# Experts and feed-forward in one block, output copies ahead of the logarithm, late weight pieces split in other steps

## The chip, the cores and the metric

The program runs on one core of one Trainium2 chip. The time is the device time of one execution in microseconds (us). A core has five engines with instruction queues of their own: TensorE (PE: matrix products and transposes; its weight loads are listed as PEld), VectorE (DVE), ScalarE (ACT), GpSimd (POOL) and SyncE (SP), which here issues nearly all data transfers.
## The reference

```python
x = attention(q, k, v)          # causal, window 128, linear bias; 4 x 576 tokens, 8 heads x 64
x = moe(x, w_skip, w_gate, w1, w2)   # top expert of 8; x + gate * (relu(x @ w1[e]) @ w2[e])
h = x @ w_in                    # 2304 x 512 times 512 x 2048
sp = np.where(h > 20.0, h, np.log1p(np.exp(np.minimum(h, 20.0))))
g = h * np.tanh(sp)
return (g @ w_out).astype(np.float32)   # 2304 x 2048 times 2048 x 512
```

## The kernel before

Three parts follow each other, each in a block of its own: `attention`, `experts` and `feed_forward`. At a block's end every engine waits for all others before it goes into the next block. `feed_forward` takes SBUF and PSUM only after `experts` has given its own back.

**Experts.** Tokens that go to the same pair of experts are gathered by GpSimd from `tokens` in DRAM, 128 rows (a job) at a time, and written back the same way. Of one job, `one` on TensorE does the hidden products (L1046), transposes and output products (L1064) into `ps_y`; VectorE's `scale_y` (L975) makes `y_sb`, and GpSimd's `put` (L763) scatters it. Behind the last job TensorE waits for `y_scaled` and does 20 warming products (`keep_warm`, L84 and L1093, two passes each); VectorE has six weight pieces of the feed-forward to split (`low_parts`, L961); GpSimd waits for its last scatter (L816). Weights are split because each product is made from three: the float32 matrices are held as a high part (`hi`, rounded) and the rest (`lo`), as are tokens and activations.

**Feed-forward.** The 2304 tokens are taken in six chunks of 384 (three tiles of 128). Each chunk has 16 steps, one for each 128 columns of the 2048 hidden ones. `step` exists once for each engine and is written out by hand; the order of the calls in it is the order on the engine. In step f:

- TensorE does `hidden` of step f (12 products, L1366) and then `output` of step f - 3 (9 products, L1383, into three PSUM banks `ps_o`, one for each token tile, over all 16 steps). So the last `output` of a chunk stands in step 2 of the next, and the first of the next chunk in its step 3.
- VectorE caps the hidden values (`u_sb`, L1313), makes `g` of step f - 2 (`n_sb`, L1317), two operations for step f - 1 (L1322, L1324), and the polynomial `n_sb` of step f (L1330).
- ScalarE takes an exponential (L1264), rounds `g` to `g_hi` (L1270), takes a logarithm (L1275) and a second exponential (L1277).
- GpSimd makes `g_lo` (L1236), for which `output` waits, and the ratio (L1230).

In steps 3, 6, 9 and 12 (`AHEAD`) TensorE also transposes a quarter of the next chunk (L1352), ScalarE rounds it to `xt_hi` (L1258) and VectorE makes `xt_lo` (L1304). In chunk 0, eight late weight pieces of 256 columns are split too: `SPLIT` gives for ScalarE's step f the piece whose high part it makes (L1284), and VectorE makes its low part one step later (L1338). When a chunk's last `output` is done, ScalarE copies the three banks to `o_sb` (L1292), at the end of that step; SyncE stores them (L1204). TensorE's first `output` of the next chunk waits for the copy of each bank.

The first tokens come by three loads (L1208), one for each tile, at the start of the block, followed by the two late weight loads (L1210). TensorE transposes them as they arrive (L1403), into `ps_o` and `ps_xt`.

Of the kernel before, what the change touches and what calls it, by code (L numbers as in the profile page):

```python
# [24 lines left out]
P = 128  # L25
# [546 lines left out]
def experts(nc, ctx, dram, ffn, cst):  # L572
# [8 lines left out]
    FB = F1 // P  # L581
    w_sb = sb("w_sb", [P, 4 * KD * F1])
# [81 lines left out]
    block = ctx.enter_context(nc.Block())  # L664
# [43 lines left out]
    def _(sp):  # L708
# [11 lines left out]
        for p in range(2, PH):  # L720

            done = jobs_of(sp, p - 2)
            sp.wait_ge(y_ready[p - 2], done)
# [4 lines left out]
    def _(pool):
# [87 lines left out]
        pool.wait_ge(y_scattered[PH - 1], before * 16)  # L816

# [177 lines left out]
    def _(pe):  # L995
# [96 lines left out]
        pe.wait_ge(y_scaled[PH - 1], totals[PH - 1])  # L1092
        keep_warm(nc, ps_y[0], cst, 20)  # L1093

def feed_forward(nc, ctx, dram, ffn, cst, out):
# [19 lines left out]
    SPLIT = {f: f - 1 for f in range(1, 1 + MINI)}  # L1116
# [43 lines left out]
    block = ctx.enter_context(nc.Block())  # L1160
# [35 lines left out]
    def _(sp):  # L1196
# [54 lines left out]
    def _(act):  # L1251
# [8 lines left out]
        def step(c, f, par):  # L1260
# [4 lines left out]
            if t2.exists():  # L1265
# [4 lines left out]
                nc.scalar.activation(g_hi[:, t2.r], n_sb[:, t2.f % NB], ACT.Copy).then_inc(g_hi_ready, 1)  # L1270
            if t.exists():
# [14 lines left out]
            if o.exists() and o.f == FT - 1:  # L1286

                for i in range(CT):
                    act.wait_ge(*((o_ready, o.c * (CT - 1) + i + 1) if i < CT - 1 else (g_used, o.s + 1)))
                    if i == 0 and (not isinstance(o.c, int) or o.c >= 1):  # L1290
                        act.wait_ge(o_stored, o.c * 16)
                    nc.scalar.activation(o_sb[:, i], ps_o[i][:, :], ACT.Copy).then_inc(o_copied, 1)  # L1292
# [120 lines left out]
def program(nc, dram, out):  # L1413
    with ExitStack() as ctx:
# [86 lines left out]
```

## Time and profile before

| | us |
|---|---|
| Median of three runs | 819.0 |
| Lowest and highest | 814.56, 819.47 |
| The profiled execution | 817.42 |
| Its span, first to last instruction | 815.6 |
| TensorE, VectorE, ScalarE, GpSimd busy | 782.9, 497.4, 366.0, 352.3 |
| Feed-forward, first transposes to the end | 377.2 to 815.6 |

The times below are in us from the start of the span. In a timeline, a row of several equal instructions (x3) gives their common length; what stands in brackets is how long the engine had been idle before and what ended this. The ends of matrix products are modelled, so a product that follows another closely starts before the other's listed end.

### The profile page before, as it was taken

To read this page: it belongs to the slowest core of one execution; us is meant where nothing else is said; L and a number is where in the kernel's file an instruction comes from. 1 tells how busy PE (TensorE), PEld (TensorE's weight loads), DVE (VectorE), ACT (ScalarE), POOL (GpSimd) and SP (SyncE) were. 2 spreads that over 40 slices of the span, in tenths; PEclk is the share of its full clock that TensorE was granted. 3 is DMA by queue.
4 is the path that set the end of the run, shared out by engine and by line. 5 is a ranking of instruction groups with operands and counts; after the bars stand their busy time and mean duration, and the time that the engine had idled before them with its cause. 6 is when DMAs were issued, how large, how long until landed. Compare 5 with 4: busy or idle time off the path is not lost.

```text
span 815.6 us, 13948 instructions
## 1 busy us (share of the span) xinstructions
PE 782.9 (96%) x4708; PEld 594.2 (73%) x4708; DVE 497.4 (61%) x878; ACT 366.0 (45%) x881; POOL 352.3 (43%) x447
## 2 busy tenths in 40 slices
PE   8999999998999999997899999999999999999996
PEld 4787788877333333337788898888888988888995
DVE  3666666665111111334888878777877787786784
ACT  4667777620101010442554545555454445455443
POOL 3555555511111021000455556555655655565654
PEclk9999999999999999998999999999999999999999
DMA  5566888610789175004001010110100001001001
GB/s 201 173 187 190 287 274 262 194 39 16 258 291 341 62 280 204 8 14 134 0 1 40 0 40 0 39 40 1 40 21 17 5 33 39 0 0 40 0 1 40
DMA packets 50325, 77.78 MB, mean 95 GB/s; under 512 B 22083, under 2 KB 23363, under 8 KB 50240
## 3 DMA queue, kind: packets, MB, share of 16 engines
q1 hardware_dynamic: 48656, 72.19, 26.8%
q0 software_dynamic: 1600, 4.70, 1.5%
q8 instruction: 40, 0.66, 0.3%
q14 instruction: 29, 0.24, 0.1%
HBM read 65.36 MB, written 12.32 MB: 95 GB/s over the span
## 4 chain that ended last, share of the span: by engine, by line
PE 42%; DVE 5%; issue 3%; ACT 1%; POOL 1%; DMA 0%; POOLq 0%; SPq 0%; ACTq 0%; DVEq 0%
PE ffn_h L1366 21%; PE ffn_o L1383 20%; DVE n_sb L1330 1%; POOL n_sb L1230 1%; DVE u_sb L1313 1%; DVE ffn_lo L1338 1%; DVE n_sb L1317 1%; DVE u_sb L1322 1%; PE ffn_xt L1352 1%; ACT r_sb L1275 1%; DMA x_sb<-tokens 0%; POOL g_lo L1236 0%; ACT o_sb L1292 0%; DVE r_sb L1324 0%; ACT xt_hi L1258 0%
## 5 line engine op out<-in xcount | busy, mean ns | idle before, releaser
L1236 POOL TENSOR_TENSOR g_lo<-n_sb,g_hi 128x384 fp32r<-128x384 f32 x96 | 119.7, 1247 | 179.4 <-ACT g_hi L1270 179.4
L1230 POOL TENSOR_TENSOR n_sb<-n_sb,r_sb 128x384 f32<-128x384 f32 x96 | 125.5, 1307 | 20.6 <-DVE r_sb L1324 20.6
L1366 PE MATMUL ffn_h<-xt_hi,ffn_lo 128*128 128x384 f32 x384 | 132.9, 346 | 0.5 <-DVE xt_lo L1304 0.5
L1275 ACT ACTIVATE r_sb<-n_sb,all_consts 128x384 f32<-128x384 f32 x96 | 59.3, 618 | 164.1 <-DVE n_sb L1330 164.1
L1366 PE MATMUL ffn_h<-xt_lo,ffn_hi 128*128 128x384 f32 x384 | 130.7, 340 | 0.0
L1366 PE MATMUL ffn_h<-xt_hi,ffn_hi 128*128 128x384 f32 x384 | 130.7, 340 | 0.0
L1383 PE MATMUL ffn_o<-ffn_hi,g_lo 128*128 128x512 f32 x288 | 116.0, 403 | 13.1 <-POOL g_lo L1236 7.0
L1330 DVE SCALAR_TENSOR_TENSOR n_sb<-u_sb 128x384 f32<-128x384 f32 x96 | 125.8, 1311 | 1.5 <-ACT u_sb L1264 1.5
L1383 PE MATMUL ffn_o<-ffn_lo,g_hi 128*128 128x512 f32 x288 | 114.5, 397 | 0.0
L1383 PE MATMUL ffn_o<-ffn_hi,g_hi 128*128 128x512 f32 x288 | 113.6, 395 | 0.0
L1313 DVE TENSOR_SCALAR u_sb<-ffn_h 128x384 f32<-128x384 f32 x96 | 53.2, 554 | 48.1 <-PE ffn_h L1366 48.1
L366 ACT ACTIVATE probs<-ps_scores,neg_max 128x256 f32<-128x256 f32 (+2 forms) x160 | 66.7, 427 | 30.0 <-DVE neg_max L407 30.0
L1366 PEld LDWEIGHTS ffn_h<-xt_hi,ffn_lo 128*128 128x128 f32 x384 | 72.9, 190 | 4.4 <-DVE xt_lo L1304 0.9
L1366 PEld LDWEIGHTS ffn_h<-xt_lo,ffn_hi 128*128 128x128 f32 x384 | 72.9, 190 | 3.2
L1383 PEld LDWEIGHTS ffn_o<-ffn_hi,g_lo 128*128 128x128 f32 x288 | 54.3, 188 | 28.3 <-issue 13.2
L1366 PEld LDWEIGHTS ffn_h<-xt_hi,ffn_hi 128*128 128x128 f32 x384 | 72.7, 189 | 0.0
L1264 ACT ACTIVATE u_sb<-u_sb 128x384 f32<-128x384 f32 x96 | 50.1, 522 | 40.3 <-DVE u_sb L1313 39.3
L407 DVE TENSOR_REDUCE neg_max<-ps_scores 128x2 f32<-128x512 f32 (+2 forms) x80 | 43.6, 578 | 36.8 <-PE ps_scores L506 36.2
L1383 PEld LDWEIGHTS ffn_o<-ffn_hi,g_hi 128*128 128x128 f32 x288 | 54.1, 188 | 13.2
L1383 PEld LDWEIGHTS ffn_o<-ffn_lo,g_hi 128*128 128x128 f32 x288 | 54.1, 188 | 8.5
L1317 DVE SCALAR_TENSOR_TENSOR n_sb<-n_sb,ffn_h 128x384 f32<-128x384 f32 x96 | 52.5, 547 | 9.1 <-POOL n_sb L1230 9.1
L1324 DVE SCALAR_TENSOR_TENSOR r_sb<-u_sb,r_sb 128x384 f32<-128x384 f32 x96 | 53.6, 558 | 3.3
(154 smaller groups left out, 1243.9 us busy)
## 6 DMA issues: line engine op xcount, KB each, us to landing
experts_even<-in_w SPq DMA_DIRECT2D x8, 2048.0 KB, 10.9
w_sb<-in_w SPq DMA_DIRECT2D x8, 2048.0 KB, 11.9
ffn_raw<-in_w_ffn SPq DMA_DIRECT2D x16, 512.0 KB, 5.5
q_raw<-in_qT SPq DMA_DIRECT2D x16, 288.0 KB, 3.8
k_raw<-in_kT SPq DMA_DIRECT2D x16, 288.0 KB, 4.3
v_sb<-in_v SPq DMA_DIRECT2D x16, 256.0 KB, 2.7
tokens<-x_out SPq DMA_DIRECT2D x64, 64.0 KB, 3.5
x_sb<-tokens SPq DMA_DIRECT2D x5, 768.0 KB, 4.7
```

The lines of the kernel that those rows point to most:

```text
L366: e = nc.scalar.activation(probs[0:n, r, h, 0:w], ps_scores[t.ring][0:n, h, 0:w], ACT.Exp, bias=neg_max[0:n, r, h:h + 1], scale=-1.0, accu ...
L407: nc.vector.tensor_reduce(neg_max[0:n, r], ps_scores[t.ring][0:n, :, 0:w], AX_X, ALU.min).then_inc(max_ready, 1)
L1230: nc.gpsimd.tensor_tensor(n_sb[:, f % NB], n_sb[:, f % NB], r_sb[:, f % 2], ALU.mult).then_inc(ratio_ready, 1)
L1236: nc.gpsimd.tensor_tensor(g_lo[:, f % 2], n_sb[:, f % NB], g_hi[:, f % 2].bitcast(F32), ALU.subtract).then_inc(g_lo_ready, 1)
L1264: nc.scalar.activation(u_sb[:, t.r], u_sb[:, t.r], ACT.Exp).then_inc(u_ready, 1)
L1275: nc.scalar.activation(r_sb[:, t.r], n_sb[:, t.f % NB], ACT.Ln, bias=cst["two"]).then_inc(ln_ready, 1)
L1313: v.tensor_scalar(u_sb[:, t.r], ps_h[t.f % HB][:, 0:C], 20.0, None, ALU.min).then_inc(min_ready, 1)
L1317: v.scalar_tensor_tensor(out=n, in0=n, scalar=-1.0, in1=ps_h[t2.f % HB][:, 0:C], op0=ALU.mult, op1=ALU.mult).then_inc(g_ready, 1)
L1324: v.scalar_tensor_tensor(out=r, in0=u, scalar=2.0, in1=r, op0=ALU.subtract, op1=ALU.mult).then_inc(b_ready, 1)
L1330: v.scalar_tensor_tensor(out=n_sb[:, t.f % NB], in0=u_sb[:, t.r], scalar=2.0, in1=u_sb[:, t.r], op0=ALU.add, op1=ALU.mult).then_inc(n_read ...
L1366: m = nc.tensor.matmul(ps_h[t.f % HB][:, 0:C], ffn[a][:, at:at + P], b[:, t.par, k], start=(n == 0), stop=(n == 3 * KD - 1))
L1383: m = nc.tensor.matmul(ps_o[i][:, :], a[:, t.r, P * i:P * i + P], ffn[b][:, at:at + D], start=(t.f == 0 and n == 0), stop=(t.f == FT - 1 a ...
```

## The change

1. `experts` and `feed_forward` share one block. Nothing waits for all engines between them any more. The feed-forward's tensors are put by address into the room of `w_sb` (from `home` on), and its PSUM banks are those of `experts`: its `ps_h` are `ps_xt` and `ps_ht` of the experts, its `ps_xt` is their `ps_h0`, its `ps_o` are their `ps_h1`, `ps_y0` and `ps_y1`; in rows of the changed kernel these older names stand. SyncE waits for the last scatter itself, ahead of the first token load; GpSimd's wait for it goes. The 20 warming products go to `ps_h[0]` and wait for nothing.
2. In ScalarE's `step` the three output copies stand ahead of the logarithm instead of behind everything.
3. `SPLIT` has the pieces in ScalarE's steps 1, 3, 4, 6, 7, 9, 10 and 12 instead of 1 to 8, and so in VectorE's steps 2, 4, 5, 7, 8, 10, 11 and 13 instead of 2 to 9.

```diff
-def experts(nc, ctx, dram, ffn, cst):
+def experts(nc, ctx, block, dram, ffn, cst):
...
+    home = -(-nc.sbuf_base // 32) * 32
...
-    block = ctx.enter_context(nc.Block())
...
-        pool.wait_ge(y_scattered[PH - 1], before * 16)
-
...
-        pe.wait_ge(y_scaled[PH - 1], totals[PH - 1])
-        keep_warm(nc, ps_y[0], cst, 20)
...
+        keep_warm(nc, ps_h[0], cst, 20)
+
+    banks = [b[:].rearrange("p a b -> p (a b)") for b in ps_xt + ps_ht] + [b[:] for b in ps_h + ps_y]
+    return {"home": home, "banks": banks, "y_scattered": y_scattered[PH - 1], "jobs_of": jobs_of}
...
+def feed_forward(nc, ctx, block, own, dram, ffn, cst, out):
...
+    place = [own["home"]]
...
-        return ctx.enter_context(nc.sbuf_tensor(name, shape, dt))
+        at = place[0]
+        place[0] += 4 * math.prod(shape[1:])
+        return nc.alloc_sbuf_tensor_at(name, shape, dt, offset=at)
...
-    SPLIT = {f: f - 1 for f in range(1, 1 + MINI)}
+    SPLIT = {f: n for n, f in enumerate((1, 3, 4, 6, 7, 9, 10, 12))}
...
+    banks = own["banks"]
+    ps_h, ps_xt, ps_o = banks[0:HB], banks[HB], banks[HB + 1:]
...
+        sp.wait_ge(own["y_scattered"], own["jobs_of"](sp, PH - 1) * 16)
+        settled(sp, cst)
         for i in range(CT):
             sp.dma_start(x_sb[:, i], dram["x"][P * i:P * i + P]).then_inc(tile_loaded[i], 16)
...
+            if o.exists() and o.f == FT - 1:
+
+                for i in range(CT):
+                    act.wait_ge(*((o_ready, o.c * (CT - 1) + i + 1) if i < CT - 1 else (g_used, o.s + 1)))
+                    if i == 0 and (not isinstance(o.c, int) or o.c >= 1):
+                        act.wait_ge(o_stored, o.c * 16)
+                    nc.scalar.activation(o_sb[:, i], ps_o[i][:, :], ACT.Copy).then_inc(o_copied, 1)
             if t.exists():
                 act.wait_ge(n_ready, t.s + 1)
...
-            if o.exists() and o.f == FT - 1:
...
-                    nc.scalar.activation(o_sb[:, i], ps_o[i][:, :], ACT.Copy).then_inc(o_copied, 1)
...
-            experts(nc, part, dram, ffn, cst)
-        with ExitStack() as part:
-            feed_forward(nc, part, dram, ffn, cst, out)
+            block = part.enter_context(nc.Block())
+            own = experts(nc, part, block, dram, ffn, cst)
+            feed_forward(nc, part, block, own, dram, ffn, cst, out)
```

SyncE at the seam, before and then changed: the last weight loads of the experts, and the first loads of the feed-forward. Semaphores waited for stand in brackets.

```order
L715 DMA w_sb<-in_w 128x8x512 [waits w1_loaded3]
L715 DMA w_sb<-in_w 128x8x512
L1439 UNCONDITIONAL_BRANCH
L1195 UNCONDITIONAL_BRANCH [waits barrier_Pool_Activation_PE_DVE_SP_release]
L1208 DMA x_sb<-tokens 128x512 x3
L1210 DMA ffn_raw<-in_w_ffn 128x1024 x2
```

```order
L716 DMA w_sb<-in_w 128x8x512 [waits w1_loaded3]
L716 DMA w_sb<-in_w 128x8x512
L1197 UNCONDITIONAL_BRANCH
L677 TENSOR_LOAD jobs_i
L677 ISA x2
L1209 REGISTER_ALU
L1212 DMA x_sb<-tokens 128x512 [waits y_scattered3]
L1212 DMA x_sb<-tokens 128x512 x2
L1214 DMA ffn_raw<-in_w_ffn 128x1024 x2
```

The wait for all engines is gone, and the first load waits for the scatters of the last phase.

ScalarE in step 2 of a later chunk, before and then changed:

```order
L1264 ACTIVATE u_sb<-u_sb 128x384 [waits min_ready]
L1270 ACTIVATE g_hi<-n_sb 128x384 [waits g_lo_ready,g_used,g_ready]
L1275 ACTIVATE r_sb<-n_sb,all_consts 128x384 [waits ratio_ready,n_ready]
L1277 ACTIVATE r_sb<-r_sb 128x384 [waits ln_ready]
L1289 ISA
L1292 ACTIVATE o_sb<-ffn_o 128x512 [waits o_stored,o_ready]
L1289 REGISTER_ALU
L1292 ACTIVATE o_sb<-ffn_o 128x512 [waits o_ready]
L1292 ACTIVATE o_sb<-ffn_o 128x512 [waits g_used]
```

```order
L1268 ACTIVATE u_sb<-u_sb 128x384 [waits min_ready]
L1274 ACTIVATE g_hi<-n_sb 128x384 [waits g_lo_ready,g_used,g_ready]
L1278 ISA
L1281 ACTIVATE o_sb<-ps_h 128x512 [waits o_stored,o_ready]
L1278 REGISTER_ALU
L1281 ACTIVATE o_sb<-ps_y 128x512 [waits o_ready]
L1281 ACTIVATE o_sb<-ps_y 128x512 [waits g_used]
L1286 ACTIVATE r_sb<-n_sb,all_consts 128x384 [waits ratio_ready,n_ready]
L1288 ACTIVATE r_sb<-r_sb 128x384 [waits ln_ready]
```

The copies now stand between `g_hi` and the logarithm, with the same waits.

VectorE in chunk 0, before and then changed, the end of step 3 (with transposes) and the step behind it:

```order
L1304 TENSOR_TENSOR xt_lo<-ffn_xt,xt_hi 128x384 [waits xt_hi_ready]
L1338 TENSOR_TENSOR ffn_lo<-ffn_raw,ffn_hi 128x256 [waits w_hi_ready]
L1313 TENSOR_SCALAR u_sb<-ffn_h 128x384 [waits b_ready,ffn_h_ready]
L1317 SCALAR_TENSOR_TENSOR n_sb<-n_sb,ffn_h 128x384 [waits ratio_ready]
L1322 SCALAR_TENSOR_TENSOR u_sb<-n_sb,r_sb 128x384 [waits r_ready]
L1324 SCALAR_TENSOR_TENSOR r_sb<-u_sb,r_sb 128x384 [waits a_ready]
L1330 SCALAR_TENSOR_TENSOR n_sb<-u_sb 128x384 [waits g_lo_ready,u_ready]
L1338 TENSOR_TENSOR ffn_lo<-ffn_raw,ffn_hi 128x256 [waits w_hi_ready]
```

```order
L1308 TENSOR_TENSOR xt_lo<-ps_h,xt_hi 128x384 [waits xt_hi_ready]
L1317 TENSOR_SCALAR u_sb<-ps_xt 128x384 [waits b_ready,ffn_h_ready]
L1321 SCALAR_TENSOR_TENSOR n_sb<-n_sb,ps_ht 128x384 [waits ratio_ready]
L1326 SCALAR_TENSOR_TENSOR u_sb<-n_sb,r_sb 128x384 [waits r_ready]
L1328 SCALAR_TENSOR_TENSOR r_sb<-u_sb,r_sb 128x384 [waits a_ready]
L1334 SCALAR_TENSOR_TENSOR n_sb<-u_sb 128x384 [waits g_lo_ready,u_ready]
L1342 TENSOR_TENSOR ffn_lo<-ffn_raw,ffn_hi 128x256 [waits w_hi_ready]
```

The piece behind `xt_lo` has gone from here; the same happens at steps 6 and 9, and the plain steps 10, 11 and 13 have a piece that they had not.

## Rows read from the trace of the kernel before

**Rows 1.** Waits of TensorE, 375-815 us: waiter, releaser, total us, times, longest.

```profile
PE ffn_o L1383 <- POOL g_lo L1236: 7.0, 6, 1.5
PE ffn_o L1383 <- ACT o_sb L1292: 4.7, 5, 1.0
PE ffn_o L1403 <- DMA x_sb<-tokens: 3.7, 2, 3.0
```

**Rows 2.** Timeline, 366-381 us: start, duration, engine, line, [idle before, releaser].

```profile
366.51 6.89 DVE L961 TENSOR_TENSOR ffn_lo<-ffn_raw,ffn_hi 128x1024 fp32r<-128x1024 f32 x6
366.64 7.57 PE L84 MATMUL ps_y<-all_consts 128*128 128x216 f32 x40 [0.85 <-DVE y_sb L975]
367.48 1.09 POOL L763 DMA_INDIRECT tokens<-y_sb,scatter_list  x1 [12.01 <-DVE y_sb L975]
374.45 1.29 SPq L1208 DMA_DIRECT2D x_sb<-tokens  x3
377.17 0.52 PE L1403 MATMUL ffn_o<-all_consts,x_sb 128*128 128x128 f32 x3 [2.96 <-DMA x_sb<-tokens]
379.11 0.90 PE L1403 MATMUL ffn_o<-all_consts,x_sb 128*128 128x128 f32 x3 [0.71 <-DMA x_sb<-tokens]
380.76 0.69 PE L1366 MATMUL ffn_h<-xt_hi,ffn_lo 128*128 128x384 f32 x1 [0.53 <-DVE xt_lo L1304]
```

**Rows 3.** GpSimd's timeline: scatter before; windows: length, busy times, clock, DMA.

```profile
352.31 1.08 POOL L763 DMA_INDIRECT tokens<-y_sb,scatter_list  x1 [13.36 <-DVE y_sb L975]
355.29 0.18 POOL L755 COPY scatter_list<-job_entry 128x1 int32<-128x1 int32 x1 [1.90 <-DMA tokens<-y_sb,scatter_list]
369.00:369.50 0.50, 0.50 (x5) 0.50 (x4) 0.50 (x1) 0.00 (x0) 0.00 (x0) 1.00 0.52 189
```

**Rows 4.** Windows, VectorE's timeline, chain of waits: the first hidden products.

```profile
379.00:379.50 0.50, 0.39 (x2) 0.39 (x3) 0.00 (x0) 0.00 (x0) 0.00 (x0) 0.50 1.31 311
385.00 0.56 DVE L1313 TENSOR_SCALAR u_sb<-ffn_h 128x384 f32<-128x384 f32 x1 [2.91 <-PE ffn_h L1366]
434.94 2.11 PE ffn_h L1366 x12
```

**Rows 5.** The timeline of ScalarE and TensorE round the first chunk boundary.

```profile
463.90 0.53 ACT L1270 ACTIVATE g_hi<-n_sb 128x384 fp32r<-128x384 f32 x1
464.52 0.39 PE L1383 MATMUL ffn_o<-ffn_hi,g_hi 128*128 128x512 f32 x1
466.25 0.62 ACT L1275 ACTIVATE r_sb<-n_sb,all_consts 128x384 f32<-128x384 f32 x1 [1.83 <-DVE n_sb L1330]
467.33 1.55 ACT L1292 ACTIVATE o_sb<-ffn_o 128x512 f32<-128x512 f32 x3
467.96 0.50 PE L1383 MATMUL ffn_o<-ffn_hi,g_lo 128*128 128x512 f32 x1 [0.93 <-ACT o_sb L1292]
```

**Rows 6.** Timeline and chain, chunk 0: VectorE's late pieces; output products.

```profile
399.94 0.42 DVE L1338 TENSOR_TENSOR ffn_lo<-ffn_raw,ffn_hi 128x256 fp32r<-128x256 f32 x1
403.53 1.23 DVE L1338 TENSOR_TENSOR ffn_lo<-ffn_raw,ffn_hi 128x256 fp32r<-128x256 f32 x1
417.97 0.47 PE L1383 MATMUL ffn_o<-ffn_hi,g_lo 128*128 128x512 f32 x1 [1.19 <-POOL g_lo L1236]
432.61 0.47 PE L1383 MATMUL ffn_o<-ffn_hi,g_lo 128*128 128x512 f32 x1 [1.20 <-POOL g_lo L1236]
445.82 2.21 PE ffn_o L1383 x9
```

**Rows 7.** The timeline and a window of the experts' start: a clock fall.

```profile
203.30 0.66 PE L1017 MATMUL ps_xt<-all_consts,x_in 128*128 128x128 f32 x4 [1.29 <-DMA x_in<-tokens,job_entry]
205.00:206.00 1.00, 1.00 (x4) 0.24 (x2) 0.00 (x0) 0.00 (x0) 0.00 (x0) 0.50 0.01 4
```

**Rows 8.** The timeline of a later chunk, after a step with transposes.

```profile
571.70 1.30 POOL L1236 TENSOR_TENSOR g_lo<-n_sb,g_hi 128x384 fp32r<-128x384 f32 x1 [2.87 <-ACT g_hi L1270]
573.14 0.47 PE L1383 MATMUL ffn_o<-ffn_hi,g_lo 128*128 128x512 f32 x1
```

More of the change, by code:

```diff
@@ L10 @@
 import functools
+import math
 from contextlib import ExitStack
@@ L1091, in _ @@
                                                       done_before=totals[p - 1] if p else None))
-        pe.wait_ge(y_scaled[PH - 1], totals[PH - 1])
-        keep_warm(nc, ps_y[0], cst, 20)
-def feed_forward(nc, ctx, dram, ffn, cst, out):
+        keep_warm(nc, ps_h[0], cst, 20)
[3 more added lines that the diff above has]
+    place = [own["home"]]
     def sb(name, shape, dt=F32):
-        return ctx.enter_context(nc.sbuf_tensor(name, shape, dt))
+        at = place[0]
+        place[0] += 4 * math.prod(shape[1:])
+        return nc.alloc_sbuf_tensor_at(name, shape, dt, offset=at)
     def sem(name):
@@ L1131, in feed_forward @@
     o_sb = sb("o_sb", [P, CT, D])
-    ps_h = [ctx.enter_context(nc.psum_tensor(f"ffn_h{i}", [P, 512], F32)) for i in range(HB)]
-    ps_xt = ctx.enter_context(nc.psum_tensor("ffn_xt", [P, 512], F32))
-    ps_o = [ctx.enter_context(nc.psum_tensor(f"ffn_o{i}", [P, D], F32)) for i in range(CT)]
+    banks = own["banks"]
+    ps_h, ps_xt, ps_o = banks[0:HB], banks[HB], banks[HB + 1:]
     first_xt = ps_o + [ps_xt]
@@ L1159, in feed_forward @@
     o_stored = sem("o_stored")
-    block = ctx.enter_context(nc.Block())
     ident = cst["ident"]
@@ L1285, in step @@
                                      ACT.Copy).then_inc(cst["w_hi_ready"], 1)
-            if o.exists() and o.f == FT - 1:
[L1288 to L1291, printed above, removed]
-                    nc.scalar.activation(o_sb[:, i], ps_o[i][:, :], ACT.Copy).then_inc(o_copied, 1)
         for k in range(KD):
```

## The prediction

> **What bounds the kernel now.** I read the waits of TensorE first, since the chain of waits runs through its two lines of the feed-forward almost to the end. From 375 us on TensorE is idle for few reasons only [rows 1]: 7.0 us for `g_lo` (six waits), 4.7 us for the output copies `o_sb` (five waits, one for each chunk boundary), 3.7 us for the first token tiles. So a change pays here exactly where it removes one of these waits, or shortens the seam between experts and feed-forward. The seam stands in the timeline [rows 2]: TensorE waits 0.85 us for VectorE's last `y_sb`, does 40 warming products in 7.57 us, to 374.21, and only then the block ends; SyncE starts the token loads at 374.45. GpSimd's last scatter had been issued at 367.48. The first tile reaches TensorE at 377.17, the third at 379.11, the first product of the feed-forward starts at 380.76.
>
> **Part 1, one block.** The loads wait for the scatter alone. When has it landed? The trace doesn't show this wait, but the scatter before gives its length [rows 3]: issued at 352.31, and GpSimd, which waits for it, goes on at 355.29, 2.98 us later. By that the last one has landed at 367.48 + 2.98 = 370.46. It also shows in the DMA share, 0.52 in the half microsecond from 369.0 and so over by about 369.5; landing can be some 0.3 us earlier than 370.46, and hardly later. Queued behind SyncE's new wait are the three token loads, the two late weight pieces and the load of chunk 1, nothing else; the weight loads of the experts are ahead of it. All of them start 374.45 - 370.46 = **4.0 us** earlier, and so does everything behind them if nothing else is late. What could be late: the warming products no longer wait for `y_sb`, so they run from 366.64 - 0.85 = 365.79 to 373.36, and the first tile arrives at 377.17 - 4.0 = 373.2, so TensorE just goes over from one to the other. VectorE's six `ffn_lo` pieces end at 366.51 + 6.89 = 373.40 [rows 2]; its first `xt_lo` is due three tiles later, after 375. Bounds: 1.0 us if SyncE gets away only when VectorE's pieces are through (373.4), 4.9 us if it could go as soon as the data have moved (369.5); I take the value of the earlier scatter, the same operation beside the same kind of VectorE work. What SyncE adds, a register load of the job count, is done long before, while it would wait anyway: nothing.
>
> **Part 1, the clock.** TensorE was idle for 2.96 us before the first tile and 0.71 us before the third [rows 2], and its granted clock, 1.00 before, is 0.50 from about 379 us (1.2 instead of 2.4 GHz) [rows 4]. The first block of twelve hidden products starts at 380.76, and VectorE takes its result at 385.00: 4.24 us; at the full clock the same twelve take 2.11 us [rows 4]. All that comes behind (the exponential, the logarithm, the first `g_lo`) hangs on this first block. After the change TensorE has no gap of 3 us: it goes from the warming products into the first transposes, waits at most 0.7 us for the third tile and 0.5 us for `xt_lo`. I take it that the clock stays up: **2.1 us** more. Bounds: 0 if it falls all the same, 2.3 us with the last transposes at full clock too.
>
> **Part 2, copies ahead of the logarithm.** At the first boundary [rows 5] ScalarE is done with `g_hi` at 464.43, then idle for 1.83 us until VectorE's `n_sb` lets the logarithm start at 466.25; the copies come behind it, at 467.33, and TensorE waits 0.93 us for the first of them (467.96). The last product of the chunk ends at 464.91. Moved ahead, the three copies of 0.52 us (1.55 in all) start at 464.43; the third has to wait for the product's end and starts at 465.4 anyway, ends at about 466.0, 0.25 us before the logarithm can start. So what now stands behind the waiting copies, logarithm and second exponential, is not delayed, and all three buffers are free a microsecond before TensorE wants the first, at 467.03. The five waits of [rows 1] go: **4.7 us**. What is late next is `g_lo`: it had been late by nothing at these places, and the exponential that the copies held back comes earlier too. The price on the other side: at this place `n_sb` ran without GpSimd beside it, and will run beside it as elsewhere, which by the two durations of `ffn_lo` [rows 6] costs VectorE some 0.8 us once a chunk. Bounds: 0 (another wait in its place) to 4.7 us.
>
> **Part 3, the late pieces.** Only VectorE's half leaves the steps with transposes; ScalarE's half stays in steps 3, 6, 9 and 12. A piece of `ffn_lo` takes 0.42 us where a step has transposes (VectorE has waited for `xt_hi`, GpSimd is through) and 1.23 us in a plain step [rows 6]. That is the place where a rule speaks against the change. The Trainium skill (SBUF — State Buffer, its part on the shared port) says that a VectorE instruction with two SBUF inputs and a GpSimd instruction that reads SBUF exclude each other for a whole instruction; the two durations agree with it, and by the rule alone the three pieces that leave cheap places would cost 3 x 0.81 = 2.4 us. By the periods it is nearly nothing. In chunk 0 `g_lo` makes TensorE wait three times behind a step with transposes, the last two at 417.97 and 432.61, 14.64 us apart (one step with transposes and a piece, two plain ones with a piece); the next period, without pieces in its plain steps, is TensorE's own, 445.82 - 432.61 = 13.21 us [rows 6]. The new periods of VectorE are 14.64 - 0.42 = 14.2 us three times over: two periods and the lead-in get shorter by 0.42 each, 1.26 together, and the period from 432.61 grows from 13.21 to 14.2, by 1.0. Net gain 0.3 us at best; as starts are nearer together than durations (0.33 instead of 0.42), I take **0**, with bounds from 2.4 us lost to 1.3 us won. Three waits of 1.2 us become four of about 1 us.
>
> **The sum** is against the profiled execution, 817.4 us (span 815.6 and 1.8 around it): 817.4 - 4.0 - 2.1 - 4.7 - 0 = 806.6 us. The median of the runs, 819.0, is 1.6 above the profiled one, and the same sum from it gives 808.2. I name the middle, 807.4. What this kernel's measurement can tell from no change is about 1%, 8.2 us.
>
> **The rivals.**
> A, the forecast, 10.8 us gained. From the lowest and highest run (814.56 and 819.47) it gives 803.8 to 808.7.
> B, **the clock falls anyway**. For it: at the experts' start the clock was at 0.50 from 205 us after a gap of only 1.29 us, with transposes and a shorter gap behind it [rows 7], and the seam keeps just such a mixture of transposes and short gaps. Against it: the gaps shrink from 3.7 us to about 1.2, and in the feed-forward the waits of 0.93 us and of 1.2 us, with full work on both sides, don't bring the clock down (each block of hidden products behind them takes its 2.11 us). The 2.1 us stay out: 808.7 from the profiled run, 810.3 from the median. The Trainium skill (TensorE: Matmul & The Clock Gate, part 1) says that the activity monitor runs freely and does not start with the kernel, so the same kernel can change its clock at another place in another run; by it A and B could alternate between runs of one program. No row here shows that.
> C, **the scatter takes longer than I think**, because VectorE's pieces hold GpSimd's port: the loads then start at about 373.4, gain 1.0 us, with an idle TensorE and a fallen clock. 817.4 - 1.0 - 4.7 = 811.7, or 813.3. Against it the DMA share of 0.52 at 369 us, in the middle of these pieces [rows 3].
> D, **the copies only exchange one wait for another**: the removed 0.93 us comes back as a wait for `g_lo`, since behind a step with transposes `g_lo` is ready at 573.0, and TensorE takes it at 573.14 [rows 8]. Gain 6.1 us: 811.3, or 812.9. Against it: that tightness is at steps 6, 9 and 12, which TensorE's own pace sets and which all move together.
> E, **slower**: the same 0.1 us of slack. If VectorE and GpSimd fall out of step through the third of a chunk that now runs denser, `g_lo` is late in each group of three steps, as in chunk 0, at 1.2 us a time; chunks 1 to 4 have four such groups each. 16 x 1.2 = 19.2 us: 825.8, or 827.4. It needs VectorE's three steps to grow past TensorE's 13.2 us, and without pieces they take 11.8 (14.64 - 0.42 - 2 x 1.23). It decides from 10.8 us on, nine such waits.
> That the change does not do what it says holds for ScalarE's half of part 3, and is in the sum.
>
> **Chances.** A 0.76, B 0.12, C 0.03, D 0.05, E 0.04. The range from 803.2 to 812.2 holds A, B and most of C and D. Faster by over 1% (below 810.8): nearly all of A (0.69; the rest for medians that wander by as much as the runs before do) and half of B (0.07), 0.76. Within 1%: 0.07 + 0.05 + 0.08 = 0.20. Slower: 0.04.
>
> **What would show it.** The token loads start within 3.5 us of the last scatter's issue; TensorE's idle time before its first tile is under 0.5 us; the granted clock is 1.00 through the first hidden products, and the first `u_sb` comes 2.2 us after the first of them. No wait of `ffn_o` for `o_sb` is left, the copies stand between `g_hi` and the logarithm, and each later chunk is 0.93 us shorter. In chunk 0 `g_lo` is waited for four times instead of three behind a step with transposes. I am wrong if the clock shows 0.50 after the seam, if the waits for `g_lo` in chunks 1 to 4 are more than none, or if chunk 0, from the first `u_sb` to the first output product of chunk 1, changes by over 1 us beside the copies' 0.93.

## The result, and the profile after

| | median us | lowest to highest | runs |
|---|---|---|---|
| Before | 817.56 | 814.56 to 821.71 | 6 |
| Changed | 808.03 | 804.30 to 809.86 | 6 |

The ratio is 0.9876, with a 95% interval of 0.9837 to 0.9914: 1.2% faster. It is worked out from the runs and is not quite the quotient of the two medians, 0.9884; the same holds for the ratios below. The forecast was 807.4. The profiled execution took 807.18 us with a span of 805.3, 10.3 us less than before (815.6).

First the waits of TensorE of the changed kernel from 365 to 815 us (total, times, longest), to be read against [rows 1]:

```profile
PE ps_h L1387 <- POOL g_lo L1240: 6.8, 7, 1.4
PE ps_h L1407 <- DMA x_sb<-tokens: 1.8, 1, 1.8
PE ps_h L1387 <- issue: 1.8, 1, 1.8
PE ps_xt L1370 <- DVE xt_lo L1308: 0.8, 1, 0.8
```

No wait for `o_sb` is left. Two waits for token tiles have become one.

The timeline of the changed kernel round the seam, GpSimd, SyncE, TensorE and VectorE in turn (VectorE's first row is its six weight pieces), and two windows of the first hidden products (after the length, busy times of PE, PEld, DVE, ACT, POOL, then granted clock, DMA share, GB/s). They answer to [rows 2] and [rows 4]:

```profile
367.42 1.09 POOL L763 DMA_INDIRECT tokens<-y_sb,scatter_list  x1 [12.00 <-DVE y_sb L973]
...
369.97 1.29 SPq L1212 DMA_DIRECT2D x_sb<-tokens  x3
371.31 0.91 SPq L1214 DMA_DIRECT2D ffn_raw<-in_w_ffn  x2
...
365.66 7.57 PE L85 MATMUL ps_h<-all_consts 128*128 128x216 f32 x40
373.06 0.27 PE L1407 MATMUL ps_h<-all_consts,x_sb 128*128 128x128 f32 x1
...
375.99 0.33 PE L1407 MATMUL ps_h<-all_consts,x_sb 128*128 128x128 f32 x1 [1.81 <-DMA x_sb<-tokens]
...
377.49 0.45 PE L1370 MATMUL ps_xt<-xt_hi,ffn_lo 128*128 128x384 f32 x1 [0.85 <-DVE xt_lo L1308]
...
366.45 6.89 DVE L959 TENSOR_TENSOR ffn_lo<-ffn_raw,ffn_hi 128x1024 fp32r<-128x1024 f32 x6
...
379.91 0.56 DVE L1317 TENSOR_SCALAR u_sb<-ps_xt 128x384 f32<-128x384 f32 x1 [1.08 <-PE ps_xt L1370]
...
378.00:379.00 1.00, 1.00 (x7) 1.00 (x6) 0.83 (x2) 0.00 (x0) 0.00 (x0) 1.00 0.28 84
379.00:380.00 1.00, 1.00 (x7) 1.00 (x7) 0.09 (x1) 0.00 (x0) 0.00 (x0) 1.00 0.99 387
```

The last scatter is issued at 367.42, as before (367.48), so the two traces can be laid over each other here. The token loads start 2.55 us behind it instead of 6.97. The transposes follow the warming products without a gap. The clock is 1.00, and the first `u_sb` comes at 379.91 instead of 385.00: the seam has given 5.1 us.

The first chunk boundary of the changed kernel, ScalarE, then TensorE, then SyncE's store of the chunk and of the next one, against [rows 5]:

```profile
459.17 0.53 ACT L1274 ACTIVATE g_hi<-n_sb 128x384 fp32r<-128x384 f32 x1
459.60 0.58 ACT L1281 ACTIVATE o_sb<-ps_h 128x512 f32<-128x512 f32 x1
460.08 1.07 ACT L1281 ACTIVATE o_sb<-ps_y 128x512 f32<-128x512 f32 x2
461.53 0.62 ACT L1286 ACTIVATE r_sb<-n_sb,all_consts 128x384 f32<-128x384 f32 x1 [0.37 <-DVE n_sb L1334]
...
462.15 0.40 PE L1387 MATMUL ps_h<-ffn_hi,g_lo 128*128 128x512 f32 x1
...
461.40 0.41 SPq L1206 DMA_DIRECT2D out<-o_sb  x1
530.59 0.39 SPq L1206 DMA_DIRECT2D out<-o_sb  x1
```

The copies end at 461.15, the logarithm still waits 0.37 us for VectorE, and TensorE goes straight on at 462.15. The two stores are 69.19 us apart. In the kernel before they are

```profile
469.12 0.41 SPq L1204 DMA_DIRECT2D out<-o_sb  x1
539.37 0.39 SPq L1204 DMA_DIRECT2D out<-o_sb  x1
```

70.25 us apart. Over the four stores of the first chunks it is 70.28 and 69.18 us a chunk, so a removed wait is worth 1.10 us there. Five of these would give 5.5; the fifth, into the last chunk, was longer than the others (1.02 us listed instead of 0.93), and all five together give 5.7 (below, p2_copies). Chunk 0 has paid 0.4 us for the pieces (below): 5.1 + 5.7 - 0.4 = 10.4 us, beside 10.3 in the spans.

### The profile page after: what moved, and what is told of

Same layout as the page of the kernel before. It is cut to its first block, busy times and chain, and to the rows that moved or that the text cites. A ratio compares the mean times of both kernels' runs of the same rounds, so it can differ in the third digit from the quotient of the medians.

```text
span 805.3 us, 13940 instructions
## 1 busy us (share of the span) xinstructions
PE 779.5 (97%) x4708; PEld 591.5 (73%) x4708; DVE 502.8 (62%) x878; ACT 366.0 (45%) x881; POOL 355.5 (44%) x447
## 4 chain that ended last, share of the span: by engine, by line
PE 63%; DVE 7%; issue 3%; DMA 1%; ACT 1%; POOL 1%; POOLq 0%; SPq 0%; DVEq 0%
PE ps_y L1387 14%; PE ps_xt L1370 11%; PE ps_ht L1370 10%; PE ps_y L1062 9%; PE ps_h L1044 9%; PE ps_h L1387 7%; DVE ffn_lo L1342 1%; DVE h_sb L952 1%; DVE n_sb L1334 1%; DVE u_sb L1317 1%; PE ps_ht L1051 1%; POOL n_sb L1234 1%; DVE n_sb L1321 1%; DVE u_sb L1326 1%; PE ps_h L1008 1%
## 5 line engine op out<-in xcount | busy, mean ns | idle before, releaser
L1387 PE MATMUL ps_y<-ffn_lo,g_hi 128*128 128x512 f32 x192 | 76.4, 398 | 0.0
L1387 PE MATMUL ps_y<-ffn_hi,g_lo 128*128 128x512 f32 x192 | 75.9, 395 | 0.0
L1387 PE MATMUL ps_y<-ffn_hi,g_hi 128*128 128x512 f32 x192 | 75.9, 395 | 0.0
L1370 PE MATMUL ps_xt<-xt_hi,ffn_lo 128*128 128x384 f32 x192 | 66.0, 344 | 0.8 <-DVE xt_lo L1308 0.8
L1370 PE MATMUL ps_ht<-xt_hi,ffn_lo 128*128 128x384 f32 x192 | 65.9, 343 | 0.0
L1370 PE MATMUL ps_xt<-xt_lo,ffn_hi 128*128 128x384 f32 x192 | 64.9, 338 | 0.0
L1370 PE MATMUL ps_xt<-xt_hi,ffn_hi 128*128 128x384 f32 x192 | 64.9, 338 | 0.0
L1370 PE MATMUL ps_ht<-xt_hi,ffn_hi 128*128 128x384 f32 x192 | 64.9, 338 | 0.0
L1370 PE MATMUL ps_ht<-xt_lo,ffn_hi 128*128 128x384 f32 x192 | 64.9, 338 | 0.0
L1326 DVE SCALAR_TENSOR_TENSOR u_sb<-n_sb,r_sb 128x384 f32<-128x384 f32 x96 | 52.8, 550 | 0.3 <-ACT r_sb L1288 0.3
```

The lines of the kernel that those rows point to most:

```text
L1326: v.scalar_tensor_tensor(out=u, in0=n, scalar=2.0, in1=r, op0=ALU.add, op1=ALU.mult).then_inc(a_ready, 1)
L1370: m = nc.tensor.matmul(ps_h[t.f % HB][:, 0:C], ffn[a][:, at:at + P], b[:, t.par, k], start=(n == 0), stop=(n == 3 * KD - 1))
L1387: m = nc.tensor.matmul(ps_o[i][:, :], a[:, t.r, P * i:P * i + P], ffn[b][:, at:at + D], start=(t.f == 0 and n == 0), stop=(t.f == FT - 1 a ...
```

## The experiments

All twelve kernels were timed beside the kernel before on their chip. Since the time before the seam wanders from run to run (last section), the profiled runs are compared by what comes **behind the issue of the last scatter**, in us:

| kernel | median us | ratio, 95% interval | token loads | first hidden product | first u_sb | end of span |
|---|---|---|---|---|---|---|
| before | 817.56 | 1 | 6.97 | 13.28 | 17.52 | 448.1 |
| changed | 808.03 | 0.9876 (0.9837-0.9914) | 2.55 | 10.07 | 12.49 | 437.9 |
| p1_one_block | 811.04 | 0.9892 (0.9842-0.9942) | 2.55 | 9.05 | 11.47 | 442.2 |
| p2_copies | 811.29 | 0.9905 (0.9872-0.9937) | 6.98 | 13.99 | 18.24 | 443.1 |
| p3_split | 819.61 | 1.0008 (0.9983-1.0033) | 6.98 | 12.77 | 17.01 | 448.4 |
| p12_old_split | 806.39 | 0.9838 (0.9787-0.9890) | 2.54 | 8.91 | 11.33 | 436.3 |
| no_warm | 808.83 | 0.9889 (0.9849-0.9929) | 2.55 | 10.34 | 14.59 | 439.9 |
| weights_behind | 806.36 | 0.9849 (0.9810-0.9888) | 2.56 | 8.67 | 11.09 | 436.4 |
| weights_ahead | 808.12 | 0.9879 (0.9842-0.9915) | 4.57 | 10.71 | 14.95 | 440.2 |
| late_at_seam | 801.26 | 0.9814 (0.9769-0.9859) | 4.68 | 10.22 | 12.63 | 433.5 |
| cheap_places | 807.14 | 0.9842 (0.9786-0.9899) | 2.56 | 9.00 | 12.69 | 435.9 |
| one_load_early | 803.80 | 0.9805 (0.9764-0.9847) | 3.19 | 9.39 | 11.82 | 432.8 |
| warm_between | 802.53 | 0.9790 (0.9748-0.9831) | 2.97 | 9.50 | 11.93 | 432.9 |
| warm_routing | 800.78 | 0.9798 (0.9773-0.9824) | 2.98 | 9.55 | 11.97 | 433.0 |

**Each part alone, and the first two together.** p1_one_block is the changed kernel with the old `SPLIT` and the copies in their old place, p12_old_split the changed kernel with the old `SPLIT` alone. p2_copies and p3_split are the kernel before with one part each (in all code below, `...` stands for lines left out):

```diff
 p2_copies
             nc.scalar.activation(g_hi[:, t2.r], n_sb[:, t2.f % NB], ACT.Copy)...
+            if o.exists() and o.f == FT - 1:
+                ...
...
-            if o.exists() and o.f == FT - 1:
-                ...
 p3_split
-    SPLIT = {f: f - 1 for f in range(1, 1 + MINI)}
+    SPLIT = {f: n for n, f in enumerate((1, 3, 4, 6, 7, 9, 10, 12))}
```

> The change's first part alone: one block for experts and feed-forward, output copies and late pieces as in the kernel before. My account of the two traces: the seam is worth 5.1 us (first u_sb at 379.9 instead of 385.0), nothing else moves, so the whole is 5.1 us below the kernel before (about 812.5), the five waits of 0.93 us for o_sb are all there, and chunk 0 from the first u_sb to the first output product of chunk 1 takes 82.96 us as before. The rival, that the parts need each other (an earlier seam is given back later, since chunk 0 is bound by VectorE), would show less than 4 us gained, or chunk 0 longer than 83.3 us.

> The second part alone: the output copies ahead of the logarithm, everything else as in the kernel before. If a removed wait is worth 1.09 us, as the chunk periods of the two traces say (70.27 and 69.19), five of them are worth 5.4 us (about 812.2) and each later chunk takes 69.2 us. If it is worth the 0.93 us that the waits list, it is 4.7 us (812.9) and 69.34 us a chunk. If it takes a new wait in exchange, g_lo is waited for in chunks 1 to 4 and the gain is under 3 us.

> The third part alone: only the steps in which late pieces are split are changed. My account by periods: four waits for g_lo, periods of 14.30 us, 0.2 us slower than before (817.8), which is no difference in the time but shows in chunk 0: 83.2 us from the first u_sb to the first output product of chunk 1, against 82.96. The rival that takes the words of the change at face value (a piece costs least where there are no transposes) wants 3 x 0.33 = 1.0 us less; the rival that counts durations (three pieces from 0.42 to 1.23 us) wants 2.4 us more.

> The change without its third part: one block and early copies, late pieces in steps 1 to 8 as before. If the parts add up (5.1 + 5.4 us) it is 10.5 us below the kernel before, 0.2 us below the changed kernel, and has three waits for g_lo in chunk 0 behind steps with transposes instead of four. If the third part was needed for the others, it is slower than the changed kernel (808) by 1 us or more.

Measured: 0.9892, 0.9905, 1.0008 and 0.9838. The block alone brings the first `u_sb` 6.05 us nearer to the scatter (17.52 - 11.47) and the end 5.9 us, more than the 5.1 expected, since its third tile came sooner than the changed kernel's; the copies alone bring the end 5.0 us nearer, although their third tile came 0.7 us later than in the kernel before. From the first output product to the end of the span, which leaves the seam out, it is 422.5 us in the kernel before and 416.8 in p2_copies: the five waits were worth 5.7 us. Both parts together bring the end 11.8 us nearer; 5.9 and 5.0 make 10.9, and that later tile is 0.7 of the difference. So the two gains add up within 0.2 us; they lie at different places. The five waits for `o_sb` stand in p1_one_block and p3_split with the same 4.7 us as before, and are gone in the other two. Part 3 alone is no gain: the interval of its ratio holds 1.

What part 3 does shows in TensorE's timeline of chunk 0. First p1_one_block (old table), then p3_split (new table), then the changed kernel; each TensorE row is a wait behind a step with transposes, the one below it the next such wait. The VectorE row is one of the pieces in a plain step:

```profile
398.11 0.47 PE L1387 MATMUL ps_h<-ffn_hi,g_lo 128*128 128x512 f32 x1 [1.26 <-POOL g_lo L1240]
412.75 0.47 PE L1387 MATMUL ps_h<-ffn_hi,g_lo 128*128 128x512 f32 x1 [1.20 <-POOL g_lo L1240]
```

```profile
417.02 0.47 PE L1383 MATMUL ffn_o<-ffn_hi,g_lo 128*128 128x512 f32 x1 [0.86 <-POOL g_lo L1236]
431.32 0.47 PE L1383 MATMUL ffn_o<-ffn_hi,g_lo 128*128 128x512 f32 x1 [0.86 <-POOL g_lo L1236]
```

```profile
398.10 1.23 DVE L1342 TENSOR_TENSOR ffn_lo<-ffn_raw,ffn_hi 128x256 fp32r<-128x256 f32 x1
...
412.21 0.47 PE L1387 MATMUL ps_h<-ffn_hi,g_lo 128*128 128x512 f32 x1 [0.85 <-POOL g_lo L1240]
426.50 0.47 PE L1387 MATMUL ps_h<-ffn_hi,g_lo 128*128 128x512 f32 x1 [0.86 <-POOL g_lo L1240]
440.80 0.47 PE L1387 MATMUL ps_h<-ffn_hi,g_lo 128*128 128x512 f32 x1 [0.86 <-POOL g_lo L1240]
```

In the kernel before, the product that answers to the last row waited for nothing:

```profile
445.69 0.47 PE L1383 MATMUL ffn_o<-ffn_hi,g_lo 128*128 128x512 f32 x1
```

The period of three steps falls from 14.64 to 14.30 us, and there are four of these waits instead of three. From the first output product of chunk 0 to the first of chunk 1 it is 74.88 us in the kernel before and in p1_one_block, 75.26 in p3_split; with the copies moved, to the first store, 73.03 in p12_old_split and 73.41 in the changed kernel. Twice the same 0.38 us lost. That the changed kernel's median lies 1.6 us above that of p12_old_split is not all part 3: in its profiled run the third tile also came 1.2 us later behind the scatter. No comparison in one set of runs splits the rest.

**Is the clock the 2 us?** The change without its warming products:

```diff
-        keep_warm(nc, ps_h[0], cst, 20)
```

> The changed kernel without its 20 warming products: TensorE is idle for some 7 us at the seam. This prices the clock. My account: the clock falls to 0.50 as before the change, the first twelve hidden products take 4.2 us instead of 2.3, the first u_sb comes about 2 us later after the scatter's issue (14.3 us instead of the 11.3 to 12.5 of the three one-block runs), and nothing else moves: 2 us slower than the changed kernel, about 810. The rival, that the early loads alone make the gain of the seam and the clock is nothing, wants the same time as the changed kernel.

Measured: 808.83, 0.9889. TensorE's and VectorE's timeline, and two windows:

```profile
372.89 0.45 PE L1406 MATMUL ps_h<-all_consts,x_sb 128*128 128x128 f32 x1 [7.16 <-DMA x_sb<-tokens]
376.12 0.47 PE L1406 MATMUL ps_h<-all_consts,x_sb 128*128 128x128 f32 x1 [1.29 <-DMA x_sb<-tokens]
377.76 0.69 PE L1369 MATMUL ps_xt<-xt_hi,ffn_lo 128*128 128x384 f32 x1 [0.53 <-DVE xt_lo L1307]
...
382.01 0.56 DVE L1316 TENSOR_SCALAR u_sb<-ps_xt 128x384 f32<-128x384 f32 x1 [2.91 <-PE ps_xt L1369]
...
378.00:380.00 2.00, 2.00 (x7) 2.00 (x8) 1.10 (x3) 0.27 (x1) 0.00 (x0) 0.50 0.48 104
380.00:382.00 2.00, 2.00 (x8) 2.00 (x7) 0.00 (x0) 0.00 (x0) 0.00 (x0) 0.50 0.76 293
```

The loads start as in the changed kernel, the clock is 0.50, and the first block takes 4.25 us to `u_sb` instead of 2.42. So the full clock is worth 1.8 us on that block, 2.1 with what stands ahead of it (14.59 - 12.49), and 2.0 at the end (439.9 - 437.9). The medians (808.83 and 808.03, of different sets of runs) cannot tell this apart: 2 us more had been expected, and they show 0.8.

**The order of the loads.** The two late weight loads behind the transposes; or ahead of the scatter's wait:

```diff
 weights_behind
+        sp.wait_ge(xt_ready, KD)
         for n in range(EARLY, PAIRS):
             sp.dma_start(ffn["raw"]...
-        sp.wait_ge(xt_ready, KD)
 weights_ahead
+        sp.wait_ge(own["y_scaled"], done)
...
+        for n in range(EARLY, PAIRS):
+            sp.dma_start(ffn["raw"]...
+        sp.wait_ge(own["y_scattered"], done * 16)
...
-        for n in range(EARLY, PAIRS):
-            sp.dma_start(ffn["raw"]...
```

> The changed kernel with the two late weight loads issued behind the first transposes instead of right behind the three token tiles. The third token tile reached TensorE 6.0 us after the loads' issue in the changed kernel, 4.3 to 5.4 us in the others. If the weight pieces in the same queue take its share of the transfer, it comes at 3.7 us or so here, every time, and the seam is 1 to 2 us shorter (about 806.5). If the spread is the token loads' own, the third tile stays between 4.3 and 6 us and the time is that of the changed kernel.

> The changed kernel with the two late weight loads issued ahead of the token tiles, as soon as VectorE has made the last y_sb (their room is that of x_in). They then have 3.4 us before the token loads start. If contention is what delays the third tile, it comes about 4 us after its issue; the scatter, which now shares the DMA with the weights, may land up to 1 us later than its 2.5 us. Net 0 to 1.5 us less than the changed kernel. If it's the token loads' own spread, no difference.

Measured: 806.36 and 808.12. With the weights issued later, the third tile comes 4.61 us after the issue of the loads, not the 3.7 expected; with the weights right behind it, it came after 4.29 to 6.15 us in eight profiles (before 4.66, changed 6.02), in one of them sooner than 4.61. All fourteen profiles together say more on this (last section). With the weights ahead the tile comes after 4.49, but they are in the way of the scatter itself: SyncE gets away 4.57 us behind it instead of 2.55, twice the delay that had been expected at most, and nothing is gained. And in this run the clock fell. Its SyncE and TensorE timeline and a window:

```profile
369.63 0.82 SPq L1213 DMA_DIRECT2D ffn_raw<-in_w_ffn  x2
375.00 1.28 SPq L1217 DMA_DIRECT2D x_sb<-tokens  x3
...
377.77 0.30 PE L1410 MATMUL ps_h<-all_consts,x_sb 128*128 128x128 f32 x1 [1.53 <-DMA x_sb<-tokens]
379.49 0.48 PE L1410 MATMUL ps_h<-all_consts,x_sb 128*128 128x128 f32 x1 [0.26 <-DMA x_sb<-tokens]
...
378.00:380.00 2.00, 1.56 (x11) 1.09 (x10) 0.00 (x0) 0.00 (x0) 0.00 (x0) 0.79 0.39 123
```

**The late pieces out of chunk 0 altogether.** weights_ahead, and with the weights there so early, both halves are split at the seam:

```diff
+        act.wait_ge(cst["w_loaded"], 16 * PAIRS)
+        high_parts(range(EARLY, PAIRS))
...
-        low_parts(range(8, EARLY))
+        low_parts(range(8, PAIRS))
...
-    SPLIT = {f: n for n, f in enumerate((1, 3, 4, 6, 7, 9, 10, 12))}
+    SPLIT = {}
...
```

> As weights_ahead, and the late pieces are split whole at the seam (two of 1024 columns, ScalarE at about 372, VectorE behind its six others, from 373.4 to 375.7) instead of eight small ones in chunk 0. If chunk 0 is bound by these pieces, as I hold, the waits for g_lo behind steps with transposes go (periods of 13.2 us), and from the first output product to the first store it takes 69.2 us or so instead of 73.4 (changed kernel) and 73.0 (its old steps): 4 us less, at the price of up to 0.9 us at the seam. About 804. If the waits for g_lo are those of chunk 0 for another reason (fresh pipeline, transposes), they stay and the time is that of weights_ahead.

Measured: 801.26, 0.9814, where about 804 had been expected. Its timeline, VectorE, ScalarE, TensorE, SyncE's first store:

```profile
364.72 9.16 DVE L961 TENSOR_TENSOR ffn_lo<-ffn_raw,ffn_hi 128x1024 fp32r<-128x1024 f32 x8
...
369.97 2.00 ACT L824 ACTIVATE ffn_hi<-ffn_raw 128x1024 fp32r<-128x1024 f32 x2 [12.34 <-DMA ffn_raw<-in_w_ffn]
...
375.92 0.45 PE L1375 MATMUL ps_xt<-xt_hi,ffn_lo 128*128 128x384 f32 x1 [0.84 <-DVE xt_lo L1313]
...
395.69 0.47 PE L1392 MATMUL ps_h<-ffn_hi,g_lo 128*128 128x512 f32 x1 [0.30 <-POOL g_lo L1245]
...
455.37 0.41 SPq L1208 DMA_DIRECT2D out<-o_sb  x1
```

ScalarE was idle at the seam (12.34 us) and VectorE free, since both wait for the tokens there: the first hidden product comes 10.22 us behind the scatter, 10.07 in the changed kernel, although the token loads start 2.1 us later. In chunk 0 one wait of 0.30 us behind a step with transposes is left of four; from the first output product (386.38) to the first store it takes 68.99 us instead of 73.41. So the late pieces had cost chunk 0 4.4 us in all, and both tables of part 3 only moved this about.

**The cheap places.** The opposite of part 3: VectorE's pieces two at a time into the steps with transposes, behind `xt_lo`.

```diff
-    SPLIT = {f: n for n, f in enumerate((1, 3, 4, 6, 7, 9, 10, 12))}
+    SPLIT = {f: n for n, f in enumerate((1, 2, 4, 5, 7, 8, 10, 11))}
+    LOW = {3: (0, 1), 6: (2, 3), 9: (4, 5), 12: (6, 7)}
...
-            if isinstance(c, int) and c == 0 and f - 1 in SPLIT:
+            for n in LOW.get(f, ()) if isinstance(c, int) and c == 0 else ():
...
```

> The changed kernel with VectorE's eight late pieces where they cost 0.42 us: two each behind xt_lo in the steps with transposes (3, 6, 9, 12), none in plain steps; ScalarE makes their high parts in steps 1, 2, 4, 5, 7, 8, 10 and 11. That is against the words of the third part. By my account of the periods VectorE's three steps then take 14.30 - 2 x 1.16 + 2 x 0.33 = 12.6 us, under TensorE's 13.2, and only the slack of 0.1 us behind a step with transposes is overrun: waits for g_lo of some 0.5 us at most, chunk 0 from its first output product to its first store 69.5 to 71.5 us instead of 73.4 (changed kernel) and 73.0 (its old steps). That is 2 to 4 us less than the changed kernel. If a piece costs the same wherever it stands, the periods stay at 14.3.

Measured: 807.14, 0.9842. VectorE's and TensorE's timeline:

```profile
409.07 0.56 DVE L1309 TENSOR_TENSOR xt_lo<-ps_h,xt_hi 128x384 fp32r<-128x384 f32 x1 [1.62 <-ACT xt_hi L1263]
409.54 0.75 DVE L1343 TENSOR_TENSOR ffn_lo<-ffn_raw,ffn_hi 128x256 fp32r<-128x256 f32 x2
...
413.29 0.47 PE L1388 MATMUL ps_h<-ffn_hi,g_lo 128*128 128x512 f32 x1 [0.60 <-POOL g_lo L1241]
```

Two pieces take 0.75 us here and 2.5 in plain steps (2 x 1.23). From the first output product to the first store it is 70.78 us, 2.6 less than with part 3's table; the waits for `g_lo` are 0.6 us. By its median the kernel isn't told from the changed one: in the profiled run its clock fell at the seam (0.56 from 378 to 380 us), which took 1.3 us of the gain back.

**Towards a better version.** From late_at_seam, one late weight load moved up to the phase before; then short warming products between the tiles' transposes:

```diff
 one_load_early
+        sp.wait_ge(y_scaled[PH - 2], jobs_of(sp, PH - 2))
+        sp.dma_start(ffn["raw"][:, EARLY * 1024:EARLY * 1024 + 1024], ...
...
 warm_between, beside it
+            if i:
+                keep_warm(nc, ps_h[0], cst, 3 if i == 1 else 2)
 warm_routing, beside both: fill ahead of and behind the routing's table products
-        keep_warm(nc, ps_y[0], cst, 10)
+        keep_warm(nc, ps_y[0], cst, 14)
...
-        keep_warm(nc, ps_y[0], cst, 11)
+        keep_warm(nc, ps_y[0], cst, 14)
```

> As late_at_seam, but the first late weight piece is loaded as soon as the last phase but one is through (its room, slots 0 and 1 of x_in, is free then), so that only one load of 512 KB goes beside the last scatter instead of two. In late_at_seam the token loads started 4.7 us after the scatter's issue instead of 2.55. If the two loads did that by sharing the transfer, it is 3.6 us or less here, and the first u_sb comes 1 us earlier after the scatter's issue (11.6 instead of 12.6): about 800. If the scatter waits for something else, it stays at 4.7.

> As one_load_early, with three warming products behind the second token tile's transposes and two behind the third's, into a bank that nothing uses yet. The clock fell in one of six runs that had one block and warming products (weights_ahead), at 2 us a time. If short gaps between transposes let it fall, it stays at 1.00 here and the lowest and highest run lie closer; the median gains 0.3 us or so over one_load_early. If the products are in the way of the third tile, the first u_sb is up to 1 us later.

> This is the kernel with short products between the tile transposes of the seam, and beside that 14 instead of 10 and 11 pairs of idle-filling products in the routing stage, ahead of the table products and behind them. If the spread of the runs comes from a clock that falls after TensorE's idle time of 1.86 us there, the clock stays 1.00 from 180 to 200 us, the first gather on GpSimd stands at 197.6 to 198.3 us (197.56 and 198.13 in the two runs whose clock did not fall there, 202.6 and 202.9 in the runs where it stayed low longest), the last scatter at about 365.5 us, and the median is 2 to 3 us under that of the kernel without the longer fill, about 799.5 us. Rival: the longer fill stands in the way of the table products, or the clock falls all the same; then the first gather is at 199.7 to 203 us as in the other runs, and the median stays at about 802.5 us or rises by up to 1 us.

Measured: 803.80, 802.53 and 800.78. With 512 KB instead of 1 MB beside it SyncE gets away 3.0 to 3.2 us after the scatter's issue instead of 4.68, but the first hidden product comes only 0.7 to 0.8 us nearer. one_load_early had been expected at about 800; what lies behind the scatter gained 0.7 us, and the rest of the miss is ahead of it. Behind the scatter these three and late_at_seam are the same within 0.7 us (432.8 to 433.5); what differs between them in the medians is the stage before. warm_routing has the lowest median of the study and beats the kernel before and the changed one, whose interval lies wholly above its own (0.9773 to 0.9824); from one_load_early, warm_between and late_at_seam its ratio doesn't tell it apart. Its clock did what was expected (1.00 from 174 to 210 us, first gather at 197.77). Its median lies 1.8 us under that of warm_between, where 2 to 3 had been expected; but the kernel before was 1.0 us faster in this set of runs too, and by the two ratios (0.9798 and 0.9790) no gain is shown.

## Why the prediction was right

**Part 1, the loads: right in its mechanism, its term 0.8 us too large.** The scatter's length (2.98 us by the earlier scatter) was in fact 2.55, so the loads started 4.4 us earlier against the scatter, not 4.0. But the chain does not end there: the first tile no longer counts (TensorE is in the warming products until 373.06), the third does, and it came 6.02 us after the issue where 4.66 had been taken over from the kernel before. So the first hidden product came 3.2 us earlier against the scatter (13.28 - 10.07). Rival C is out: SyncE's loads went off at 369.97, in the middle of VectorE's pieces (366.45 to 373.34).

**The clock: right as forecast, and B was real.** The wait for the third tile was 1.81 us where I had allowed 0.7, and the clock stayed up all the same. The term for it was 2.1 us and measured 1.8 on the block; the two terms of part 1 together were 6.1 and gave 5.1 in this profile. In the three other kernels with the same seam they gave 6.05 and 6.2 and, in cheap_places, where the clock fell, 4.8. In the eight profiled runs with one block and its 20 warming products, but none between the tiles, the clock fell in two, weights_ahead and cheap_places. In cheap_places TensorE had idled for 0.81 and 0.84 us there, less than the changed kernel's 1.81 and 0.85, and up to this place both kernels have the same instructions. So that the clock held in the profiled run of the change is in part luck. How often it fell in the change's other runs isn't known: they have a mean clock each (0.994 to 0.998), and no trace. The Trainium skill (TensorE: Matmul & The Clock Gate, part 1) has the monitor run freely, so that one kernel can change its clock at different places in different runs; the traces agree as far as one profile of each kernel can show it.

**Part 2: right, undersized.** 5.7 us instead of 4.7. The idle time that a timeline lists begins at the modelled end of the product before, and matrix products overlap (the hidden products round 461 us start 0.18 us apart and are listed with 0.34 us each): the distance of starts gives 1.10 us a chunk for a listed wait of 0.93. Rival D is out: no `g_lo` wait came in the place. Rival E is out too: chunks 1 to 3 take 69.16 to 69.19 us, and no `g_lo` wait stands in chunks 1 to 4.

**Part 3: right at 0 within its bounds, measured 0.38 us lost.** The period of 14.2 came out as 14.30, since the removed piece shortens starts by 0.34 and not 0.42. Two shorter periods and the lead-in win 1.0 us. The period behind them grew by 1.2: it was 13.08 us by the products' starts (432.61 to 445.69), and not 13.21, which was read from a piece of the chain of waits (445.82) that begins behind the product's start. The other 0.2 us stand in the two steps behind the fourth wait. The rule of the Trainium skill (SBUF — State Buffer, on the shared port) that the prediction set against the change was right in its direction, and its size, 2.4 us, was not: 0.38 us were lost. The places were the cheap ones, and with all pieces there chunk 0 is 2.6 us shorter than with the new table. The change took only three away from them.

The sum against the profiled execution was -10.8 us and came out at -10.3: errors of 1.0 us too much (part 1), 1.0 too little (part 2) and 0.4 too much (part 3). That the first two cancel, and that the median fell within 0.7 us of the forecast, is partly luck; the range didn't need it.

## What to carry to other kernels

Where two stages share a block, the next stage's loads can wait for the one transfer that they need; then look which of several arrivals now ends the wait, since it need not be the one that did before. Move an instruction ahead of one that waits for another engine anyway, and price a removed wait by the distance of starts over a period, not by the listed idle time. Work that lengthens a saturated loop belongs where its engines idle together, here at the seam, before it is worth asking in which steps of the loop it stands.

## What the runs showed of the hardware

**Most of a spread of 5 us between the profiles comes from the clock in the routing stage**, before 204 us, where TensorE has the same instructions in all these kernels but warm_routing. TensorE idles there for 1.84 to 1.86 us, up to 189.1 to 190.5 us, and then its clock falls in most of the profiles, for different times. Windows of p2_copies, of the kernel before, of warm_between and of warm_routing, with the product that ends the idle time for two of them:

```profile
190.00:194.00 4.00, 4.00 (x30) 3.31 (x30) 3.90 (x12) 0.00 (x0) 0.00 (x0) 1.00 0.00 0
```

```profile
190.16 1.19 PE L1010 MATMUL ps_h<-w_sb 128*128 128x78 f32 x8 [1.86 <-DVE w_sb L944]
...
190.00:194.00 4.00, 3.84 (x19) 3.79 (x20) 3.90 (x13) 0.00 (x0) 0.00 (x0) 0.63 0.00 0
```

```profile
190.00:194.00 4.00, 4.00 (x18) 3.93 (x18) 3.90 (x13) 0.00 (x0) 0.00 (x0) 0.50 0.00 0
198.00:202.00 4.00, 4.00 (x17) 3.88 (x17) 0.36 (x2) 0.00 (x0) 0.18 (x1) 0.50 0.00 0
```

```profile
189.27 1.12 PE L1013 MATMUL ps_h<-w_sb 128*128 128x78 f32 x8 [0.40 <-DVE w_sb L947]
...
197.77 1.24 POOL L746 DMA_INDIRECT x_in<-tokens,job_entry  x1 [1.04 <-issue]
...
190.00:194.00 4.00, 4.00 (x30) 3.31 (x30) 3.90 (x13) 0.00 (x0) 0.00 (x0) 1.00 0.00 0
```

The first gather of the experts is issued at 197.56 us in p2_copies, 199.65 in the kernel before and 202.67 in warm_between, where the clock stays at half for some 14 us. From the end of the idle time to this gather it is 8.5, 9.5 and 13.2 us in the three. From the gather to the last scatter it is 167.1 to 167.8 us in all fourteen profiles but one: in one_load_early it is 169.8, with one more fall of the clock, at 243 us. So the last scatter follows, at 365.2 to 372.7 us. Each program has one trace; of its other runs only the mean clock is known, and it goes with their time (changed: 0.998 at 804.30 us, 0.994 at 809.86). With the longer fill the idle time is 0.40 us, the clock stays up, the gather stands at 197.77, and the five runs of warm_routing lie between 800.07 and 803.62. That this narrows the spread for good five runs can't show; one of them took about 3 us longer than the other four.

**A scatter's length depends on the loads beside it**: 2.54 to 2.56 us from its issue to SyncE's next load with nothing else under way, 3.0 to 3.2 with one load of 512 KB ahead of it, 4.57 and 4.68 with two.

**The arrival of the third tile varied from 4.29 to 6.15 us after the issue of the loads** in kernels whose loads stand in the same order. The slowest of the three token loads took 3.4 to 5.2 us from its own issue to its landing in the eight profiles with 1 MB of weights right behind it, and 3.1 to 3.8 us in the six without (weights_behind 3.7, weights_ahead 3.6, late_at_seam 3.1, one_load_early 3.8, warm_between 3.8, warm_routing 3.5). So the long arrivals go together with the weights behind the tiles, by up to 1.4 us and not in every execution. Why it is 6 us in some profiles and 5 in others stays open.
